# Attention ahead of a gated MLP and experts: the loads and splits of q, k and the dense weights regrouped, and unused sink keys overwritten instead of biased

## The reference

```python
def _attn_ref(q, k, v, n_sink, window):            # (4, 8, 768, 64), n_sink 4, window 128
    scores = (1 / sqrt(64)) * q @ k.T
    keep = (pos_k < n_sink) | ((rel >= 0) & (rel < window))      # rel = pos_q - pos_k
    scores = where(keep, scores, -1e9); scores -= max(scores)
    a = exp(scores); a = a / (sum(a) + 1e-9)
    return a @ v
def _moe_ref(x, w_in, w_out):                       # 3072 tokens, 512 -> 2048 -> 512
    h = x @ w_in
    return (h * cos(h)) @ w_out
def _moe2_ref(x, modality_id, w_gate, modality_bias, w1, w2):    # 8 experts, 512 -> 1024 -> 512
    # top-1 expert by softmax of x @ w_gate + modality_bias[modality_id]; out = gate * relu(x @ w1[e]) @ w2[e]
```

## Time and profile before

| | |
|---|---|
| median of 3 runs | 1179.58 us (1178.97 to 1180.91) |
| the profiled execution | 1182.43 us, span 1180.8 us |
| PE busy over the span | 1118.2 us (95%) |
| DVE, ACT, POOL | 696.9, 463.6, 336.3 us |
| attention, about | 15 to 293 us |
| dense layer, about | 293 to 834 us |
| experts | to the end |

### The profile page before, as it was taken

The page is one execution under the profiler, slowest core; times in us unless marked ns, Lnnn a source line. Parts: engine busy times, 40 slices in busy tenths (PEclk is TensorE's granted clock), DMA queues, the critical chain, the costliest instruction groups (busy, mean ns, idle before and its releaser), DMA issues.

```text
span 1180.8 us, 19688 instructions
## 1 busy us (share of the span) xinstructions
PE 1118.2 (95%) x6168; PEld 963.6 (82%) x6169; DVE 696.9 (59%) x1529; ACT 463.6 (39%) x951; POOL 336.3 (28%) x388
## 2 busy tenths in 40 slices
PE   3999989898999999999999999999999999999996
PEld 3888878787788888888888888888889899899986
DVE  4757666666565875775775776886753222522225
ACT  3545555553543333333433433434532222421124
POOL 2888888883100000000000000050322122223112
PEclk9979999988999999999999999999999999999999
DMA  7555555561510200200200200002353111411102
GB/s 200 160 165 151 166 167 165 154 185 58 196 72 1 72 1 1 72 1 1 72 1 1 72 1 1 37 5 90 109 178 127 36 53 37 149 66 50 38 19 90
DMA packets 60685, 94.93 MB, mean 80 GB/s; under 512 B 12750, under 2 KB 41806, under 8 KB 60496
## 3 DMA queue, kind: packets, MB, share of 16 engines
q1 hardware_dynamic: 54416, 79.76, 21.6%
q0 software_dynamic: 6208, 14.40, 3.7%
HBM read 75.06 MB, written 21.69 MB: 82 GB/s over the span
## 4 chain that ended last, share of the span: by engine, by line
PE 72%; DVE 2%; issue 1%; ACT 1%; POOL 1%; DMA 0%; POOLq 0%; DVEq 0%; ACTq 0%
PE twin L1645 23%; PE twin L1733 13%; PE twin L1748 11%; PE bank L1661 11%; PE twin L1661 11%; PE bank L1699 1%; PE bank L1547 0%; DMA xg<-y_scratch,next_ids 0%; PE bank L1721 0%; DVE w_lo L1365 0%; POOL k_lo L602 0%; DMA out<-late,now_ids 0%; PE twin L1516 0%; PE bank L1554 0%; PE bank L1714 0%
## 5 line engine op out<-in xcount | busy, mean ns | idle before, releaser
L674 POOL DMA_INDIRECT list_scratch<-entry,slot_i x24 | 26.7, 1111 | 518.7 <-DVE slot_i L1316 507.5
L1645 PE MATMUL twin<-x_hi,w_hi 128*128 128x512 f32 x384 | 153.1, 399 | 2.6 <-DVE g_sb L1226 2.0
L1645 PE MATMUL twin<-x_hi,w_lo 128*128 128x512 f32 x384 | 152.7, 398 | 0.0
L1645 PE MATMUL twin<-x_lo,w_hi 128*128 128x512 f32 x384 | 152.5, 397 | 0.0
L1437 DVE SCALAR_TENSOR_TENSOR g_lo<-twin,g_hi 128x256 fp32r<-128x256 f32 x112 | 47.4, 424 | 167.3 <-ACT g_hi L935 158.0
L1733 PE MATMUL twin<-xg_hi,w_hi 128*128 128x256 f32 x448 | 127.1, 284 | 5.9 <-issue 5.9
L1733 PE MATMUL twin<-xg_lo,w_hi 128*128 128x256 f32 x448 | 126.6, 283 | 0.0
L1733 PE MATMUL twin<-xg_hi,w_lo 128*128 128x256 f32 x448 | 126.2, 282 | 0.0
L935 ACT ACTIVATE g_hi<-twin 128x256 fp32r<-128x256 f32 x112 | 43.1, 384 | 188.2 <-PE twin L1733 185.2
L772 ACT ACTIVATE probs<-twin,neg_max 128x160 f32<-128x160 f32 x192 | 66.4, 403 | 123.2 <-DVE neg_max L1059 122.7
L1516 PE MATMUL twin<-k_hi,qs 128*128 128x288 f32 (+1 forms) x192 | 78.1, 408 | 36.3 <-POOL k_lo L602 18.1
(11 more groups left out here) (211 smaller groups left out, 2715.1 us busy)
## 6 DMA issues: line engine op xcount, KB each, us to landing
raw<-w_expert SPq DMA_DIRECT2D x32, 512.0 KB
raw_q<-q_twice SPq DMA_DIRECT2D x64, 192.0 KB, 2.4
raw_k<-k_twice SPq DMA_DIRECT2D x32, 224.0 KB, 2.5
raw_k<-k_twice SPq DMA_DIRECT2D x32, 208.0 KB, 2.5
v_sb<-v_n SPq DMA_DIRECT2D x16, 384.0 KB, 3.6
xT_scratch<-x_stage SPq DMA_DIRECT2D x16, 384.0 KB, 2.8
x_raw<-xT_scratch SPq DMA_DIRECT2D x6, 1024.0 KB, 5.3
y_scratch<-y_sb SPq DMA_DIRECT2D x6, 1024.0 KB, 4.4
```

The lines of the kernel that those rows point to most:

```text
L1645: last = pe.matmul(H_BANK[f % 2][:, :], a[:, w], b[:, k, :], start=x == 0, stop=x == 3 * KD - 1)
```

## The change

- q is loaded and rounded unscaled (`qs`), and GpSimd's scaling is gone; its rest is one subtraction. Scores have their own sign. VectorE takes a maximum into `row_max`; ScalarE makes `neg_max` = -0.125 times it, one operation of two elements per step, waits for it, and the exponential has the scale 0.125.
- q and k of a pair come in 4 parts instead of 8, each with both heads' columns: 4 loads, 4 splits, 4 rests, of twice the width. `PARTS` is now `((0,), (1,), (), (2,), (), (3,))`.
- The bias product is gone. Before a k part is rounded, VectorE overwrites its sink columns from `n_sink` on with key 0 (`fill_sinks`, a masked copy in raw k), so that these columns can't raise the maximum. The fill of the first half is in VectorE's step 0 and of the second in step 4, behind the maximum; ScalarE's split of k waits for it. The probabilities of these columns are cleared where the turned sinks are copied, by a scale (`sink_on`) and in `sink_part`.
- The dense weights are no longer split half a piece per pair. `w_in` is laid out by blocks of its columns. Four pieces of 1024 columns are split in the last pair's steps (hi on ScalarE, rest on GpSimd), the twelve others in steps 0 to 11 of the first chunk on ScalarE and VectorE, in the order `ORDER`; the pieces 4 to 7 are loaded at the end of attention ahead of the second chunk's x.
- At the start VectorE makes masks before it has the configuration, and the sum columns behind the first rests.

```diff
-        PARTS = ((0, 1), (2,), (3, 4), (), (5, 6), (7,))
+        PARTS = ((0,), (1,), (), (2,), (), (3,))
+        FILLS = {0: 0, 4: 1}
+        ORDER = (0, 1, 2, 3, 8, 4, 9, 5, 10, 6, 11, 7, 12, 13, 14, 15)
...
@@ SyncE
+            def load_dense(j):
+                at_least(sp, dw_lo_made, j - 3)
+                sp.dma_start(raw[:, j % 4, :], w_dense[:, ORDER[j] * PIECE:(ORDER[j] + 1) * PIECE]).then_inc(dw_loaded[j % 4], 16)
...
-            for i in range(2):
-                load_piece(0, i)
-            for f in range(2):
-                load_later(f)
+            for j in range(4):
+                load_dense(j)
...
             stage1_over(sp)
+            for j in range(4, 8):
+                load_dense(j)
             load_chunk(1)
...
@@ GpSimd, part_rest
+                    pool.tensor_tensor(k_lo[i][:, :, cols], raw_k[:, :, cols], k_hi[i][:, :, cols].bitcast(F32), ALU.subtract).then_inc(part_lo_made, 1)
                 else:
-                    pool.tensor_scalar(raw_q[HD:, h, cols], raw_q[HD:, h, cols], -0.125, None, ALU.mult).then_inc(q_scaled, 1)
...
+                    pool.tensor_tensor(qs[i][HD:, :, cols], raw_q[HD:, :, cols], qs[i][HD:, :, cols].bitcast(F32), ALU.subtract).then_inc(part_lo_made, 1)
...
@@ ScalarE
                 if is_k:
+                    act.wait_ge(sinks_filled, 2 * (2 * it + i) + c // 2 + 1)
...
             def exponentials(it, n):
                 act.wait_ge(max_made, STEPS * it + n + 1)
+                act.activation(neg_max[:, 2 * n:2 * n + 2], row_max[:, 2 * n:2 * n + 2], ACT.Copy, scale=-0.125).then_inc(bias_made, 1)
...
+                act.wait_ge(bias_made, STEPS * it + n + 1)
...
@@ VectorE
+            def fill_sinks(it, i, half):
+
+                to = sinks_of(half)
+                shape = [P, 2, 2 - half, SINK - 1]
+                dve.wait_ge(qk_loaded[2 * half + 1], 16 * (2 * it + i) + 16)
...
+                dve.copy_predicated(to[:, :, :, 1:], mask, to[:, :, :, 0:1].broadcast_to(shape)).then_inc(sinks_filled, 1)
...
                 if n < STEPS:
                     join_scores(it, n)
+                    if n % QB in FILLS and not (last and n >= QB):
+                        fill_sinks(*after_pair(it, n // QB), FILLS[n % QB])
...
             def narrow_attention():
+                make_sink_masks()
                 first_rests()
+                make_sum_columns()
...
@@ TensorE, scores
-                    pe.matmul(to[:, h, cols], q, k_lo[par][:, h, keys], start=False, stop=False)
-                    last = pe.matmul(to[:, h, sink:sink + SINK], ident_r[:, :], sink_bias[:, :], start=False, stop=True)
+                    last = pe.matmul(to[:, h, cols], q, k_lo[par][:, h, keys], start=False, stop=True)
```

More of the change, by code:

```diff
@@ L485, in _ @@
             with sp.If(narrow == 0):
-                with sp.Fori(1, ITERS) as it:
-                    for i in range(2):
-                        load_piece(it, i)
                 sp.wait_ge(any_zeros, 3)
@@ L839, in _ @@
             with act.If(narrow == 1):
-                for c in range(8):
+                for c in range(4):
                     split_part(0, 0, c)
@@ L1161, in _ @@
                 dve.sem_inc(any_step, 1)
-                with dve.Fori(0, ITERS) as it:
-                    for i in range(2):
-                        split_piece(it, i)
+                for j in range(4):
+                    split_dense(j)
                 dve.wait_ge(any_zeros, 3)
```

234 lines of the change are left out of this document (110 added, 124 removed).

## The result

The kernel after takes 1129.03 us (median of 4 runs, 1125.61 to 1134.52), the kernel before in the same comparison 1179.28 (1177.59 to 1180.91): a ratio of 0.9578 with a 95% interval of 0.9538 to 0.9619, 50.3 us less. Forecast were 31 us less, 1149, with a range that began at 1130: right in sign and in what bounded the kernel, too small by 20 us, and the measured time lies just outside the range. Wherever a ratio is given, it leaves out executions more than 1.5% above the fastest of their kernel; only e12 (three of six) and e13 (four of six) have such, and their medians are over all six. The profiled execution took 1129.06 us with a span of 1127.4.

The account below looks back on a forecast made before the run. GpSimd was taken to bound attention, TensorE next: 13.3 + 0.7 waits + 0.4 port = 14.4 us a pair instead of 16.83, gaining 36.0 us. Less 5.2 at the start, 30.8 us gives 1149, range 1130 to 1170.

Parts of the forecast that it names:

- The bound: Attention: GpSimd has no free time and sets the pace, 16.9 us a pair summed; TensorE is the next limit.
- GpSimd's part: Attention: without q scalings and weight rests, and with joined rests, GpSimd needs 8.6 us a pair instead of 16.9.
- The bias products: TensorE in attention: dropping 12 products a pair at 0.125 us saves 1.5 us, 14.8 to 13.3.
- New and longer waits: Attention's chain from scores through join and maximum to exponential: +0.7 us a pair, bounds 0 and 1.8.
- (a) to (c): Three waits in attention: ScalarE's bias operation with x staging, joined k split, VectorE's key 0 copies; together +0.7 us a pair.
- (b): Attention, ScalarE: the joined k split takes 1.0 us ahead of the sink copies of steps 1 and 5, up to +0.5 each.
- (a): ScalarE's bias operation, 0.3 us six times a pair, mostly hidden; through the staging of x, net -0.3 to +0.5 a pair.
- The port: Attention: VectorE's key 0 copies and GpSimd's rests lock each other out; one loss in four, 0.4 us a pair, bounds 0 and 4.
- Rival 3: Attention: key 0 copies lose both port races, 3.6 us a pair; 17 us slower, 1197; chance 0.08.
- The start: Before step 6: first scores near 17, second exponential near 28, step 6 at 41 not 35.75; 5.2 us lost, bounds 2 and 8.
- rival 2: Attention: a sixth of the time stays at half clock, pace 15.7 us a pair, about 1168; chance 0.16.
- The expert stage is untouched: Expert stage, behind attention: the change does nothing there; no gain or loss was counted.

Follow-up runs that it names:

- e12: Kernel after with -0.125 moved into ScalarE's splits, no separate bias operation, k's-rest product on 64 rows, rest-times-rest left out: runs 1290 to 1347 us, ratio 1.0969.
- e13: e12 with the eight sum columns made while VectorE waits for the configuration; median not given in the text, profiled execution 23 us longer than that of e12.
- e3: Kernel before with q unscaled on GpSimd and ScalarE scaling the maximum to the bias, nothing else: 25.7 us faster, 15.17 us a pair.
- e4: Kernel after with the bias products put back, two 32-column TensorE products a step: 14.24 us a pair against 13.87; total time not given.
- e6: Kernel after without ScalarE's operation scaling the maximum, so the maximum is not subtracted: ratio 0.9490 against 0.9561, 13.34 us a pair.
- e5: Kernel after with VectorE's copies of key 0 one place later in their step: pairs alternate between 14.92 and 15.85 us; total time not given.
- e7: Kernel after with four one-input GpSimd scalings of q a pair put back, factor 1.0: undisturbed pairs 15.6 us; total time not given.
- e9: Kernel after with the bias products put back twice, 24 a pair; the second dozen seemed to cost 2.00 us; total time not given.
- e8: Kernel after with the eight sum columns made while VectorE waits for the configuration: ratio 0.9561, as the unchanged kernel after.
- e1: Kernel before plus one unused 4-byte tensor that shifts later tensors by 32 bytes: 1172.31 us against 1180.51.
- e2: Kernel after with sink_on allocated last among attention's tensors, undoing the 32-byte shift for later stages: 1138.28 us against 1129.06.
- e14: As e12, but k's-rest product uses all 128 rows, with zeros in the other 64 rows of k's rest: 1123.45 us, ratio 0.9520.

## Why the prediction was off, step by step

The forecast was 31 us and 50.3 were measured. Of the missing 19 to 20 us, 7.3 are attention's pace, 3.5 the start, and 8 to 9 the address, for which the prediction had nothing.

**The bound, right.** GpSimd 16.9 us a pair before, TensorE next. e3 shows it alone: 15.17 instead of 16.88.

**GpSimd's part, right.** Slope and joining: 8.6 us forecast. Counted are 2 x 1.824 + 2.100 + 1.967 = 7.7 us, 8.4 with four hand-overs of 0.17.

**The bias products, mis-sized.** 12 x 0.125 = 1.5 us forecast, 0.37 measured (e4). The first failing step is the reading of the earlier trace rows: the 0.14 us between the starts of two weight loads is TensorE's usual distance, with or without a bias product in it; the price is the distance from this product's start to the next, 0.02 to 0.07 us, and those rows of the kernel before were there to be read.

**New and longer waits, wrong in sign.** Forecast were +0.7 us for (a) to (c) together. Taken from the same base, 14.8 - 0.37 = 14.43, the measured 13.87 leaves -0.56 for them. The operation for the bias is +0.53 (e6), so the rest is a gain of about 1.1 us, 0.93 of it between e3 and e4. The failing step is the price of the joined splits. In (b) they could only cost ("up to +0.5 each"); in (a) the prediction did see that fewer of them stand ahead of the staging of x, but took the net of it between -0.3 and +0.5. The runs show the wait for the staging at 1.35 us a pair with eight unjoined parts (e3) and 0.2 with four joined ones. The copies of key 0 take 0.29 and 0.22 us, as forecast.

**The port, right as a mechanism, nothing in steady state.** 0.4 us was forecast, one loss in four. All copies win after the first pair: a schedule that repeats every 13.87 us repeats its races too, so the cases were none or all. The margins are 0.46 and 0.39 us. e5, e7 and e9 show the other outcome, 1.5 to 2.4 us of stall a pair. Rival 3 assumed it whole: 3.6 us, all passed on. Of 1.5 and 2.4 us 0.7 passed on, so an estimate of the worst case from these rows is 13.87 + 0.7 x 3.6 = 16.4 us a pair, without the stretches at the half clock that such a stall brings (e5: 0.5 us a pair more), about the pace of before.

**The pace.** 14.4 forecast, 13.87 measured (13.91 between the exponentials): 14.83 x (16.83 - 13.91) = 43.3 us instead of 36.0. The terms side by side, forecast and measured: bias products -1.5 and -0.37, waits +0.7 and -0.56, port +0.4 and 0. The first two errors, 1.1 and 1.3 us, have opposite signs. That the pace came out within 0.5 us is luck, not evidence for its terms.

**The start, mis-sized.** Step 6 is at 37.45 instead of 35.75: 1.7 us lost, 5.2 forecast. First scores at 18.67 (I said 17), second exponential at 26.20 (28), and from there the five steps took 11.3 us against the 13 I had left them, the old pace. In e8 the first scores were on no path that counts. Up to 1.1 us of the way to the second exponential is a port stall (the copy of 23.73), which the prediction had not put there.

**The clock, right.** From 33.3 us on no stretch of attention is below 1.00, as the forecast assumed; rival 2 needed idle stretches that the kernel after does not have. They return with a port stall (e5, e7). Up to 33.3 us both kernels run at the half clock, which the prediction did not see, since the clock column reads 1.00 there.

**"The expert stage is untouched", wrong.** Nothing in its instructions changed, and it and the dense stage gave 8 to 10 us (e1, e2), and 11.3 in the profiled pair. The omitted item was the address: the diff adds `sink_on` in front of every later tensor. Together, with the medians of e1 and e2: 43.3 - 1.7 + 8.2 to 9.2 = 49.8 to 50.8 us, against 50.3 measured.

## What to carry to other kernels

Read the diff's allocations as part of the change, and when a stage without changed instructions is faster or slower, compare the medians of one product in both traces and undo the shift alone. Price a TensorE instruction by the distance between starts of products, never of weight loads, and price operations joined on an engine by all that stood ahead of the consumer, not by the longest. Where every pair takes the same time, a port race is won always or lost always; look for the margin in the timeline, since any edit that moves a step by that much turns it over.

## What the runs showed of the hardware

- A shift of 32 bytes in SBUF, from 32 off a multiple of 64 onto one, made 256-wide products 277 instead of 281 ns (line 1733) and the kernel 8.2 us faster; 64 bytes did nothing. It isn't settled which operand matters. Line 1748 gained too (e1), 390 instead of 396 ns, although the weights that it streams did not move; line 1661 did not.
- Products of 64 rows between products of 128 rows (e12): starts 0.31 to 0.33 us apart at the full clock instead of 0.13 to 0.22, each weight load starting with its own product instead of 0.13 us ahead of it, and the half clock of the start kept until about 290 us: 28.4 us a pair there instead of 13.5 for the same work with zeros in the other rows (e14).
- The clock column can read 1.00 while every product has the length of the half clock, as long as no change has been recorded: up to 32.4 us in the kernel before, 33.3 in the kernel after, about 290 in e12. Durations of a known shape are the check.
- A masked copy on VectorE with both inputs in SBUF that starts while GpSimd runs a two-input operation ends 0.09 to 0.42 us after that operation (154 cases); one that starts ahead takes its 0.22 to 0.44 us (148 cases).
